# Ranking moved into the gated stage, last comparisons split, first table of a round added in halves

## The reference

```
attention:  8 heads of 64; each row sees the 4 sink keys and the last 128 keys;  x = softmax(q k / 8) v
gated part: y = ((x @ w_a) * (x @ w_b)) @ w_out            # 512 -> 1536 -> 512
experts:    logits = y @ w_gate                            # 1536 x 8
            all 12288 logits are taken in falling order; (token, expert) is assigned
            if the token has none yet and the expert has under 192 tokens
            out[token] = relu(y[token] @ w1[e]) @ w2[e]    # 8 experts, 512 -> 1024 -> 512
```

## Time and profile before

| what | us |
|---|---|
| median of 3 runs | 611.88 (611.64 to 612.13) |
| profiled execution, its own time | 611.83 |
| its span, first to last instruction | 610.0 |
| PE busy, share of the span | 596.4 (98%) |
| DVE busy | 416.6 (68%) |
| POOL busy | 322.3 (53%) |
| granted TensorE clock | 0.998 |

### The profile page before, as it was taken

One profiled execution on the slowest core, in us unless ns is written; L12 is line 12 of the kernel. 1 busy time (PEld: TensorE's weight loads), 2 busy tenths in 40 slices (PEclk: granted clock), 3 DMA queues, 4 the chain that ended last, 5 costly groups with the idle time before them and its releaser, 6 DMA issues.

```text
span 610.0 us, 13277 instructions
## 1 busy us (share of the span) xinstructions
PE 596.4 (98%) x4708; PEld 508.6 (83%) x4708; DVE 416.6 (68%) x1329; ACT 289.8 (48%) x692; POOL 322.3 (53%) x281
## 2 busy tenths in 40 slices
PE   8999999999999999999999999999999999999995
PEld 6777778999899899889977887777777889888894
DVE  4767661332256529998889998888957767677670
ACT  5999973332333333323322224243436765667540
POOL 8677663555455556545456662000086786667741
PEclk9999999999999999999999999999999999999999
DMA  9324291443663474465114151412569677877500
GB/s 275 118 85 155 84 329 46 123 119 105 174 173 115 128 208 139 121 166 163 38 37 155 54 190 35 157 53 94 200 229 387 211 234 252 302 262 256 165 26 27
DMA packets 85456, 94.40 MB, mean 155 GB/s; under 512 B 13808, under 2 KB 63248, under 8 KB 84752
## 3 DMA queue, kind: packets, MB, share of 16 engines
q1 hardware_dynamic: 83056, 86.86, 44.5%
q0 software_dynamic: 2048, 6.29, 3.2%
q10 hardware_dynamic: 288, 0.41, 0.2%
HBM read 87.20 MB, written 6.34 MB: 153 GB/s over the span
## 4 chain that ended last, share of the span: by engine, by line
PE 82%; DVE 13%; ACT 2%; issue 2%; DMA 0%; POOL 0%; DVEq 0%; ACTq 0%; POOLq 0%
PE bank L1419 14%; PE bank L1299 11%; PE bank L1301 11%; PE bank L1300 11%; PE bank L1518 8%; PE bank L1541 4%; PE bank L1236 4%; PE bank L1520 4%; PE bank L1286 4%; PE bank L1220 3%; DVE ge L948 2%; DVE ge L950 2%; PE bank L1312 2%; PE bank L1459 1%; DVE ge L966 1%
## 5 line engine op out<-in xcount | busy, mean ns | idle before, releaser
L548 POOL TENSOR_TENSOR wl_ab<-raw_ab,wh_ab 128x1024 fp32r<-128x1024 f32 x46 | 110.3, 2398 | 108.0 <-ACT wh_ab L663 108.0
L1299 PE MATMUL bank<-xh,wh_ab 128*128 128x384 f32 x384 | 130.6, 340 | 1.2 <-DVE hid L994 1.2
L1301 PE MATMUL bank<-xh,wl_ab 128*128 128x384 f32 x384 | 128.5, 335 | 0.0
L1300 PE MATMUL bank<-xl,wh_ab 128*128 128x384 f32 x384 | 128.4, 334 | 0.0
L663 ACT ACTIVATE wh_ab<-raw_ab 128x1024 fp32r<-128x1024 f32 x46 | 48.8, 1061 | 139.1 <-PE bank L1301 139.1
L619 POOL TENSOR_TENSOR w2l<-w_raw,w2h 128x1024 fp32r<-128x1024 f32 x32 | 75.7, 2390 | 35.9 <-DVE w1l L1105 35.7
L994 DVE TENSOR_TENSOR hid<-hid,bank 128x384 f32<-128x384 f32 x48 | 26.6, 553 | 82.9 <-ACT hid L679 82.9
L1299 PEld LDWEIGHTS bank<-xh,wh_ab 128*128 128x128 f32 x384 | 72.1, 188 | 7.9 <-issue 7.7
L1518 PE MATMUL bank<-xg,w1h 128*128 128x384 f32 x256 | 73.6, 359 | 0.8 <-issue 0.6
L1300 PEld LDWEIGHTS bank<-xl,wh_ab 128*128 128x128 f32 x384 | 72.1, 188 | 0.0
L1301 PEld LDWEIGHTS bank<-xh,wl_ab 128*128 128x128 f32 x384 | 72.1, 188 | 0.0
(11 more groups left out here) (166 smaller groups left out, 1220.7 us busy)
## 6 DMA issues: line engine op xcount, KB each, us to landing
w_sb<-in_moe_w_dram SPq DMA_DIRECT2D x8, 2048.0 KB, 8.4
w_raw<-in_moe_w_dram SPq DMA_DIRECT2D x32, 512.0 KB, 8.4
raw_ab<-in_moe_w_a_dram SPq DMA_DIRECT2D x48, 256.0 KB, 3.1
raw_ab<-in_moe_w_b_dram SPq DMA_DIRECT2D x48, 256.0 KB, 3.5
raw_out<-in_moe_w_out_dram SPq DMA_DIRECT2D x24, 256.0 KB, 2.7
lb<-logit_rows SPq DMA_DIRECT2D x4, 1536.0 KB, 6.4
v_sb<-in_v_dram SPq DMA_DIRECT2D x8, 384.0 KB
woT<-in_moe_w_outT_dram SPq DMA_DIRECT2D x1, 3072.0 KB, 11.7
```

The lines of the kernel that those rows point to most:

```text
L548: pool.tensor_tensor(wl_ab[s % 2][:, :], raw_ab[s % 3][:, :], wh_ab[s % 2][:, :].bitcast(F32), ALU.subtract).then_inc(abl_done, 1)
L1299: pe.matmul(dst, lh, rh, start=first, stop=False)
L1300: pe.matmul(dst, lh, rl, start=False, stop=False)
L1301: return pe.matmul(dst, ll, rh, start=False, stop=last)
```

## The change

1. `keys_of(first, end)` takes the six instructions of the preferences for some tiles: tiles 0 to 2 in step 25, tiles 3 to 8 behind the last comparison of step 47 and ahead of `l_copy`, tiles 9 to 11 within the last 24 groups.
2. The third comparison of step 46 stands behind `h_part(47)` instead of ahead of it.
3. `compare` is cut in two, `compare` (earlier chunks) and `compare_own`. For expert 0 of the last chunk the three `compare` come first, then the keys of tiles 9 to 11 and the first choice, then the wait for `lb`, then the three `compare_own`.
4. The first round's choice takes `key` itself (no `avail`, no `keyed`, no `cut` memset). `base_rn - parts` is computed ahead of the wait for PE's counts and `LATE` is added behind it.
5. In the first stage of a round DVE adds the tables of tiles 6 to 11 to those of tiles 0 to 5, and PE sums 6 tables instead of 12. The stages are (192, 8), (24, 8), (3, 8), (1, 3); the first grid begins at BIG - N.
6. The 432 products are dealt out anew: 44, 7, then 13 and 12 in turn ahead of the pairs (44 includes the 15 issued around the logits, as 48 did), 8 ahead of the rounds, 7, 7, 7, 12 in a round, 17 behind POS. With that 184 products stand ahead of the rounds instead of 211, and `Z_ROUNDS` becomes 11.

```diff
-    Y_PLACES = 12
-    Y_FIRST, Y_PER_PAIR, Y_BETWEEN = 48, (12, 13), 13
-    Y_AT_STAGE = [7, 6, 6, 11]
-    STAGES = [(256, 8), (32, 8), (4, 8), (1, 4)]
-    Y_ROUNDS = Y_FIRST + sum(Y_PER_PAIR) * TC * E // 4 + Y_BETWEEN
+    Y_PLACES = 17
+    Y_PAIRS, Y_BETWEEN = [44, 7] + [13, 12] * (TC * E // 4 - 1), 8
+    Y_AT_STAGE = [7, 7, 7, 12]
+    STAGES = [(192, 8), (24, 8), (3, 8), (1, 3)]
+    HALVED = 1
+    Y_ROUNDS = sum(Y_PAIRS) + Y_BETWEEN
...
+        halves = ties[:, 0:NT // 2, :, :]
...
             for s in range(STEPS):
                 h_part(s)
+                if s == STEPS - 1:
+                    compare_of_step(STEPS - 2, 2)
+                if s == 2 * NF + 1:
+                    dve.wait_ge(l_in[0], 16 * TC)
+                    keys_of(0, TC)
...
-                if s + 1 < STEPS:
+                if s + 2 < STEPS:
                     compare_of_step(s, 2)
...
             compare_of_step(STEPS - 1, 2)
+            keys_of(TC, (NC - 1) * TC)
             l_copy(NC - 1)
             dve.wait_ge(l_out, 1)
...
-            dve.wait_ge(lb_in[NC - 1], 16)
             for e in range(E):
                 for t in range(NT - TC, NT):
                     compare(t, e)
+                    if e > 0:
+                        compare_own(t, e)
+                if e == 0:
+                    keys_of(NT - TC, NT)
+                    choose(key)
+                    dve.wait_ge(lb_in[NC - 1], 16)
+                    for t in range(NT - TC, NT):
+                        compare_own(t, e)
...
+            link(dve.tensor_tensor(upper[:, :, :], base_rn[:, :, :], parts[:, :, :], ALU.subtract))
             dve.wait_ge(ge_counted, GROUPS)
-            link(dve.tensor_tensor(upper[:, :, :], LATE[:, 0:NT * E].rearrange("p (t e) -> p t e", t=NT),
-                                   base_rn[:, :, :], ALU.add))
-
-            link(dve.tensor_tensor(Rn[:, :, :], upper[:, :, :], parts[:, :, :], ALU.subtract))
-            link(dve.memset(cut[:, :], 0.0))
+            link(dve.tensor_tensor(Rn[:, :, :], upper[:, :, :], LATE[:, 0:NT * E].rearrange("p (t e) -> p t e", t=NT),
+                                   ALU.add))
...
             for r in range(E - 1):
-                choose()
+                if r > 0:
+                    choose_again()
...
+                    if i < HALVED:
+                        link(above)
+                        dve.tensor_tensor(halves[:, :, 0:m, :], atleast[:, 0:NT // 2, 0:m, :], atleast[:, NT // 2:NT, 0:m, :],
+                                          ALU.add).then_inc(atleast_ready, 1)
+                    else:
+                        above.then_inc(atleast_ready, 1)
...
-                    for t in range(NT):
+                    source, tiles = (halves, NT // 2) if i < HALVED else (atleast, NT)
+                    for t in range(tiles):
                         mm = pe.matmul(CNT[:, 0:m * E], ones16[:, :],
```

More of the change, by code:

```diff
@@ L963, in compare @@
                     dve.wait_ge(ge_counted, m - 3)
-                c, own = t // TC, P * (t % TC + 1)
+                c = t // TC
                 earlier = g[:, 0:C * c].rearrange("p (c t) -> p c t", c=c)
@@ L967, in compare, with compare_own @@
                                   accum_out=rank_parts[:, t, e, 0:1]).then_inc(ge_ready, 1)
-                dve.scalar_tensor_tensor(out=g[:, C * c:C * c + own], in0=lb[:, c, e, 0:own], scalar=li,
+            def compare_own(t, e):
+                m = group_of(t, e)
+                c, own = t // TC, P * (t % TC + 1)
+                dve.scalar_tensor_tensor(out=ge[m % 4][:, C * c:C * c + own], in0=lb[:, c, e, 0:own], scalar=L[:, t, e:e + 1],
                                          in1=OWN[:, C - own:C], op0=ALU.is_ge, op1=ALU.mult,
@@ L1001, in h_part, with link, keys_of @@
                     compare_of_step(s, 1)
+            routes = 0
+            def link(ins):
+                nonlocal routes
+                ins.then_inc(routed, 1)
+                routes += 1
+                dve.wait_ge(routed, routes)
+            def keys_of(first, end):
+                of, n = slice(first, end), end - first
+                mine = L[:, of, :].unsqueeze(3).broadcast_to([P, n, E, E])
+                other = L[:, of, :].unsqueeze(2).broadcast_to([P, n, E, E])
+                link(dve.tensor_tensor(beats[:, of, :, :], other, mine, ALU.is_gt))
+                link(dve.tensor_tensor(ties[:, of, :, :], other, mine, ALU.is_equal))
+                link(dve.tensor_tensor(ties[:, of, :, :], ties[:, of, :, :],
+                                       lower[:, :, :].unsqueeze(1).broadcast_to([P, n, E, E]), ALU.mult))
+                link(dve.tensor_tensor(beats[:, of, :, :], beats[:, of, :, :], ties[:, of, :, :], ALU.add))
+                link(dve.tensor_reduce(worse[:, of, :], beats[:, of, :, :], AX.X, ALU.add))
+                link(dve.tensor_scalar(key[:, of, :], worse[:, of, :], -1.0, float(E), ALU.mult, ALU.add))
             for s in range(STEPS):
                 h_part(s)
+                if s == STEPS - 1:
[3 more added lines that the diff above has]
+                    keys_of(0, TC)
                 if s - 1 in GATE_AT:
@@ L1019, in _, with choose, choose_again @@
             compare_of_step(STEPS - 1, 2)
+            keys_of(TC, (NC - 1) * TC)
             l_copy(NC - 1)
             dve.wait_ge(l_out, 1)
[L1023 to L1030, removed]
             def over_t(ap):
                 return ap.unsqueeze(1).broadcast_to([P, NT] + list(ap.shape[1:]))
[L1036 to L1043, removed]
-            dve.wait_ge(lb_in[NC - 1], 16)
+            def choose(of):
+                link(dve.tensor_reduce(best[:, :], of[:, :, :], AX.X, ALU.max))
+                link(dve.tensor_tensor(chosen[:, :, :], of[:, :, :],
+                                       best[:, :].unsqueeze(2).broadcast_to([P, NT, E]), ALU.is_equal))
+            def choose_again():
+                link(dve.tensor_tensor(avail[:, :, :], Rn[:, :, :], over_t(cut[:, :]), ALU.is_ge))
+                link(dve.tensor_tensor(keyed[:, :, :], avail[:, :, :], key[:, :, :], ALU.mult))
+                choose(keyed)
             for e in range(E):
@@ L1457, in _ @@
                     pe.wait_ge(atleast_ready, n)
-                    for t in range(NT):
+                    source, tiles = (halves, NT // 2) if i < HALVED else (atleast, NT)
+                    for t in range(tiles):
                         mm = pe.matmul(CNT[:, 0:m * E], ones16[:, :],
-                                       atleast[:, t, 0:m, :].rearrange("p m e -> p (m e)"),
-                                       start=(t == 0), stop=(t == NT - 1))
+                                       source[:, t, 0:m, :].rearrange("p m e -> p (m e)"),
+                                       start=(t == 0), stop=(t == tiles - 1))
                     mm.then_inc(counted, 1)
```

20 lines of the change are left out of this document (7 added, 13 removed).

## The result

| | before | after |
|---|---|---|
| median of the runs | 611.85 us | 618.51 us (617.04 to 619.11, 4 runs) |
| ratio | 1 | 1.0104 (95%: 1.0092 to 1.0116) |
| profiled execution, its span | 611.83, 610.0 | 619.11, 616.9 |
| first product of y | 313.07 | 313.34 |
| first pair counted (wait of PE ahead) | 331.29 (0) | 333.39 (2.72) |

1.04% slower; 613.8 was forecast, and the result lies outside the range of 610.3 to 615.9. The span grew by 6.9 us: 0.80 up to the first count of the rounds, 67.62 - 63.07 = 4.55 in the rounds, 4.10 - 2.75 = 1.35 from POS to the last product, 0.13 from there to the gather, and 0.07 behind it. The second and third were forecast as 4.1 and 1.4. The first was forecast as -3.5, so 4.3 us are missing there.

The account below looks back on a forecast made before the run. PE and DVE were taken to run neck and neck, with y ending the stage. -3.5 up to the first count, +4.1 in the rounds and +1.4 behind POS gave +2.0 on 611.83: 613.8 us, range 610.3 to 615.9.

Parts of the forecast that it names:

- What bounds the kernel: Up to the gather: PE and DVE run neck and neck; y, not the choice, ends the stage.
- the 0.9 us that the lists were said to have to spare: Ahead of the gather: lists of rows come later by less than their 0.9 us of slack, so the gather waits for y.
- First pair: First pair of the last 24 groups counted at 330.5 instead of 331.29, set by DVE.
- The holds by POOL: DVE's 16-bit work of tiles 9 to 11 and the choice, held by POOL: 0 to 1.7 us, taken as 0.4.
- rival 3: Ahead of the first pair: POOL holds DVE twice, 1.7 us in place of 0.4, giving 615.1; chance 0.20.
- PE's stand: Ahead of the first pair: PE arrives at 328.6 and stands 1.9 us.
- Rounds: First count of the rounds to POS: 67.2 us instead of 63.07, 4.1 more; 9.2 to 9.9 a round.
- The halves' balance of nothing: First stage of a round: halves cost DVE 0.40 and shorten the count by 0.18, so the chain isn't shortened.
- Behind POS: From POS on: 17 products instead of 11, 1.4 us more.
- Keys in step 25: Keys of tiles 0 to 2 lie in DVE's 3.6 us wait for ACT in each gated step: cost nothing.
- 1 (PE never waits): At the first pair: DVE is there by 328.6, rounds start at 368.7, 1.7 earlier, giving 612.1; chance 0.22.
- 2 (rounds at PE's pace): In the rounds: extras shrink from 3.8 to 0.9 or less, giving 610.9, or 610.0; chance 0.16.

Follow-up runs that it names:

- experiment 8: Kernel after with step 46 as before, keys of tiles 3 to 5 in step 37, 9 to 11 and first choice behind `l_copy`, whole tables, in-between deal: 614.54 us.
- experiment 11: experiment 8 with 52 products ahead of the first pair, 9 ahead of the rounds, 7, 7, 7, 11 a round, first choice in the last counts' wait: 611.55 us.
- experiment 12: experiment 11 with the keys of tiles 3 to 5 in step 27 instead of step 37: 611.36 us, ratio 0.9987 to the kernel before.
- experiment 6: Kernel after with whole tables (`HALVED = 0`), PE adding all twelve in every stage: 617.99 us.
- Experiment 4: Kernel after with eight products moved from behind POS to ahead of the first pair (52 instead of 44): 615.51 us.
- experiment 3: Kernel after with keys of tiles 9 to 11 and the first choice right behind `l_copy`: 617.17 us.
- experiment 1: Kernel before with only the new deal of the 432 products: 618.63 us.
- experiment 5: Kernel before with 12 products moved from ahead of the first pair to behind POS, DVE's work untouched: 620.19 us.
- Experiment 7: Kernel after with step 46's third comparison back ahead of `h_part(47)`: 616.21 us.
- experiment 2: Kernel after with the old deal of products: 616.16 us.
- tenth run: Kernel after with small products that compute nothing: 3 and 8 ahead of step 47's two last counts, 20 ahead of the first pair: 620.84 us.
- experiment 9: experiment 5 with ten small products that compute nothing ahead of each of the first pair's two counts: 620.81 us.

## Why the prediction was wrong

**What bounds the kernel.** Right for the two engines neck and neck. That y and not the choice ends the stretch holds for the kernel after, where the gather waits for the last store of y, but not for the kernel before: there the two are level. The prediction looked at the first list of rows (442.3); the second was ready at 443.03, and the gather started 0.17 behind that, while the last store of y, was issued at 440.8, and such a store took 2.1 to land (median). In experiments 8, 11 and 12, with nine products behind POS, the gather also starts 0.16 to 0.17 behind the second list. So the 0.9 us that the lists were said to have to spare were not there. It costs the forecast nothing, since y came late enough in the kernel after, but it limits what a still shorter deal behind POS can gain.

```profile
442.87 0.16 DVE L1127 SCALAR_TENSOR_TENSOR idx<-idx_f 64x8 int32<-64x8 f32 x1
```
```profile
442.07 0.16 DVE L1163 SCALAR_TENSOR_TENSOR idx<-idx_f 64x8 int32<-64x8 f32 x1
442.40 1.15 POOL L602 DMA_INDIRECT yg<-y_rows,idx  x1 [71.63 <-DVE idx L1163]
```

(The first row is of the kernel before, its gather in the earlier trace rows; the other two are of experiment 11.)

**First pair.** This step failed, in two of its terms.
- *The holds by POOL*, put at 0.4 of at most 1.7, measured 3.3. The prediction read the earlier trace rows as if only 16-bit instructions were held, because the f32 `ties` at 322.27 was not. But that one had begun 0.5 us before POOL's. In the rows what decides is who starts first: here an f32 `beats` and even a `key` of 24 elements were held. The rule of the skill was weighed, and put down wrongly; rival 3 was the right mechanism with half its price. The pair came at 333.39, 2.9 behind the forecast of 330.5. In the second trace of the same stretch (experiment 6) the holds were 2.3, so their size is not fixed: it hangs on when POOL starts.
- *PE's stand*, forecast as 1.9 and priced at 1.9. It was 2.72, with 0.39 + 1.13 at step 47 (1.6 forecast), and the half clock behind both was priced at nothing. From the first pair to the first count 41.3 us passed instead of 39.9: 1.4 more. Experiment 4, with the clock full there, took just the 39.9. 2.9 + 1.4 is the 4.3 that is missing. The half clock behind step 47 is hidden in the 2.9: PE came to the pair at 330.7 instead of 328.6 (328.8 in experiment 3, where the clock was full), so even with no hold at all the pair would have been at 330.7.

Experiments 1 and 5 show the stand's cost with DVE's program as before (in 5 with 1.1 us of a hold in it), and in 4 and 11 it comes back where the stand is shortened or gone, in 4 by 1.4 us. Experiment 7 shows why a small delay mattered: 1.0 us ahead of step 47's count cost 2.3. The prediction had that 1.0 and let PE's part of it hide in the later stand. But in the trace of the kernel after it also brought half pace at 322 to 326 and moved POOL's low parts by 2.3, and with these the holds of the keys grew by 1.4. The half pace there is no fixed price of the delay: the same two stands (0.4 and 1.13) were followed by it in three traces (the kernel after, 2, 6) and not in two (3, 4).

**Rounds.** Right, 4.55 for 4.1; 9.2 to 10.0 a round. The halves' balance of nothing was right (experiment 6).

**Behind POS.** Right, 1.35 for 1.4; from the last product to the gather 3.63, where it was 3.50.

**Keys in step 25** at nothing: right. The first product was 0.27 later in this trace, but at 312.94 to 312.97 in those of experiments 2, 3, 4 and 6, which have the same gated part, and at 313.07 in the kernel before.

**Rivals.** 1 (PE never waits) and 2 (rounds at PE's pace) were both refuted. The true outcome was rival 3 and a doubling that no case held; the range should have reached for it.

What stays open: why the small products of the tenth run didn't keep the clock up, and why the same stands are followed by half pace in one execution and not in another; why in experiments 2 and 4 the stores of y took about 3.0 us to land (median) instead of 2.1 to 2.4, which puts the gather 4.9 and 4.4 us behind the last product there and 3.6 in the kernel after; and the share of the holds in the time of the kernel after, apart from the stand, which no run took out alone. That the holds of the moved work alone are the loss is excluded by experiment 1, which has none of that work.

## What to carry to other kernels

Where PE is the bound and runs in program order, the filling ahead of a count must outlast the engine that feeds it: taking 16 products (3.6 us) from ahead of a count that DVE can't make earlier saved nothing here, and part of the stand was paid again in half pace (1.4 us behind 2.7). When work on DVE is moved, lay it against POOL's timeline and ask of each instruction which of the two starts first; if POOL does, price it at the rest of POOL's instruction, less 0.15 us here. Ask it again of the work behind any wait that becomes longer (experiment 5). Moving such work to a stretch in which the engine waits anyway (step 27 instead of 37) put everything behind it 1.0 us earlier. And where a kernel's runs fall into groups by mean clock, compare a trace with the run it is of, and groups of like clock with each other: 0.8 us between experiments 11 and 12 that way, 0.2 by the medians.

## What the runs showed of the hardware

- A DVE instruction on two SBUF tensors, or the `tensor_scalar` on 128x24 of f32 in SBUF, that started while POOL's two-input instruction ran ended behind it by its own unheld time less 0.14 to 0.16: 0.03 for one of 0.18, 0.11 for 0.26, 0.21 for 0.36, and 0.40 for the two of 0.56 in the earlier trace rows. So 0.18 became 1.20 and 0.26 became 1.52. POOL's of 1.30, started while `ties` of 322.27 ran, ended 1.16 behind it, which is the same sum. The comparisons (L968, one tensor; L976, the second operand in PSUM) were never held, nor the reductions, nor `Rn` where it reads PSUM (0.26 at 372.64 in experiment 8, under POOL's of 372.45).
- A stand of PE by 2.7 us in sum (1.34 + 1.34) was followed by full pace for 1.5 us, then by six products at 0.43 us each instead of 0.227. At the first pair the clock fell behind every stand of 1.54 to 3.6 us in sum (seven traces) and not behind the one of 1.00 (experiment 4). Elsewhere the same stand did both: 0.4 + 1.13 at step 47 as told above, 2.18 in the last round (0.67 at 440 to 444 in experiment 5, 1.00 in experiment 9). The Trainium skill, "TensorE: Matmul & The Clock Gate", Part 1, gives 1.2 GHz as the state behind idling, half of 2.4; the 0.43 agrees.
- Runs of one kernel can lie in groups by clock: about 1 us apart in experiments 11 and 12, with mean clocks of 0.994 and of 0.997 to 0.999, and 3.8 us apart in experiment 9, with 0.990 to 0.993 and 0.998.
